# An attention and feed-forward kernel: everything that trails the scores is put one tile later

## The reference

```python
q_bits = (einsum('bhsd,dk->bhsk', q, proj) > 0)      # proj: 64 x 6, the same for k
mask   = q_bucket[..., :, None] == k_bucket[..., None, :]
scores = where(mask, q @ k.T / 8, -1e9)
attn   = exp(scores - rowmax) / (rowsum + 1e-9)
x = (attn @ v)                                       # 2 x 8 heads, 768 tokens, 64 wide -> 1536 x 512
h = x @ w_in;  g = 0 if h <= -1, h if h >= 1, (h+1)^2/4 between;  x = g @ w_out
h = x @ w_in2; g = h - tanh(h);                                   out = g @ w_out2
```

## Time and profile before

| | |
|---|---|
| median of 3 runs | 763.33 us (761.89 to 765.22) |
| the profiled execution | 763.58 us |
| its span, first to last instruction | 761.8 us |
| granted TensorE clock | 1.000 of full speed |
| first scores (pair 0, tile 0) | 7.35 us |
| last scores (pair 7, tile 11) | 224.62 us |
| first product of the second matrix of layer 1 | 249.00 us |

### The profile page before, as it was taken

One profiled execution on the slowest core, in us unless ns is written; L12 is line 12 of the kernel. 1 busy time (PEld: TensorE's weight loads), 2 busy tenths in 40 slices (PEclk: granted clock), 3 DMA queues, 4 the chain that ended last, 5 costly groups with the idle time before them and its releaser, 6 DMA issues.

```text
span 761.8 us, 11646 instructions
## 1 busy us (share of the span) xinstructions
PE 751.5 (99%) x3712; PEld 636.7 (84%) x3712; DVE 426.3 (56%) x741; ACT 343.3 (45%) x679; POOL 290.3 (38%) x226
## 2 busy tenths in 40 slices
PE   6999999999999999999999999999999999999998
PEld 4889989989998888888888888878888888888886
DVE  5999999999994674343433677762221322232223
ACT  5789788888894323343333323242221322222222
POOL 7667977977989992000000465650000000000000
PEclk9999999999999999999999999999999999999999
DMA  6545445454324131000000123210000100010001
GB/s 207 173 129 146 122 133 143 131 127 138 109 77 149 60 134 56 1 0 1 1 0 1 55 84 111 83 56 1 1 0 1 55 0 0 0 55 1 1 0 56
DMA packets 21032, 49.48 MB, mean 65 GB/s; under 512 B 4782, under 2 KB 6958, under 8 KB 21002
## 3 DMA queue, kind: packets, MB, share of 16 engines
q1 hardware_dynamic: 20858, 48.68, 21.2%
q10 hardware_dynamic: 144, 0.39, 0.1%
HBM read 41.26 MB, written 3.19 MB: 58 GB/s over the span
## 4 chain that ended last, share of the span: by engine, by line
PE 87%; DVE 8%; ACT 3%; issue 2%; DMA 0%; DVEq 0%; ACTq 0%
PE ps L677 29%; PE ps L598 29%; PE ps L589 9%; PE ps L575 9%; DVE g_raw L913 5%; PE ps L555 4%; PE ps L562 4%; PE ps L512 2%; DVE g_mid L910 1%; ACT g_mid L781 1%; ACT g_hi L787 1%; DMA qk_raw<-qk 0%; PE ps L519 0%; DVE clamped L836 0%; DVE g_lo L921 0%
## 5 line engine op out<-in xcount | busy, mean ns | idle before, releaser
L598 PE MATMUL ps<-x_hi,w 128*128 128x512 f32 (+1 forms) x768 | 251.8, 389 | 0.0
L921 DVE TENSOR_TENSOR g_lo<-g_raw,g_hi 128x512 fp32r<-128x512 f32 x96 | 71.1, 741 | 243.5 <-ACT g_hi L787 243.5
L787 ACT ACTIVATE g_hi<-g_raw 128x512 fp32r<-128x512 f32 x96 | 60.7, 632 | 289.0 <-PE ps L677 224.1
L598 PEld LDWEIGHTS ps<-x_hi,w 128*128 128x128 f32 x768 | 144.1, 188 | 29.7
L598 PE MATMUL ps<-x_lo,w 128*128 128x512 f32 (+1 forms) x384 | 149.4, 389 | 0.0
L677 PE MATMUL ps<-g_hi,w 128*128 128x512 f32 x384 | 125.8, 389 | 0.3 <-DVE g_lo L921 0.3
L677 PE MATMUL ps<-w,g_hi 128*128 128x512 f32 x384 | 118.2, 389 | 0.0
L853 DVE TENSOR_TENSOR p_lo<-ps,p_hi 128x384 fp32r<-128x384 f32 x192 | 97.9, 551 | 11.8 <-ACT p_hi L733 11.5
L373 POOL TENSOR_SCALAR w<-stage 128x1024 fp32r<-128x1024 f32 x32 | 37.8, 1180 | 163.8 <-PE ps L677 162.8
L733 ACT ACTIVATE p_hi<-ps 128x384 fp32r<-128x384 f32 x192 | 84.3, 488 | 30.6 <-PE ps L575 29.3
L723 ACT ACTIVATE probs<-clamped,row_stats 128x768 f32<-128x768 f32 x96 | 89.6, 933 | 6.9 <-DVE clamped L836 6.7
(11 more groups left out here) (62 smaller groups left out, 858.7 us busy)
## 6 DMA issues: line engine op xcount, KB each, us to landing
stage<-weights SPq DMA_DIRECT2D x32, 512.0 KB, 3.3
qk_raw<-qk SPq DMA_DIRECT2D x15, 384.0 KB, 4.2
q_raw<-qq SPq DMA_DIRECT2D x15, 384.0 KB, 4.2
k_raw<-kk SPq DMA_DIRECT2D x15, 384.0 KB, 5.1
v_raw<-v SPq DMA_DIRECT2D x16, 192.0 KB, 3.9
inv_wide<-factors SPq DMA_DIRECT2D x16, 192.0 KB, 4.2
out<-stage SPq DMA_DIRECT2D x12, 256.0 KB, 2.1
q_a<-q_b SPq DMA_DIRECT2D x14, 192.0 KB
```

What stands on the lines that cost most here:

```text
L598: last = nc.tensor.matmul(ps[:, f % H_BANKS, :], w[:, f, wp, k * P:(k + 1) * P], xs[:, k, bass.ds(t * TOK, TOK)], start=(k == 0 and wp == ...
L787: nc.scalar.activation(g_hi[:, slot, :], g_raw[:, slot, :], ACT.Copy).then_inc(g_hi_ready, 1)
L921: nc.vector.tensor_tensor(g_lo[:, slot, :], g_raw[:, slot, :], g_hi[:, slot, :].bitcast(F32), ALU.subtract).then_inc(g_split, 1)
```

## The change

Five constants grow by one tile, the two turns in which POOL scales become 9 and 11, and the two bit products move from the ends of turns 5 and 7 to the ends of turns 6 and 8, on PE and DVE alike. No instruction is added or removed.

```diff
-TRANSPOSE_LAG = 4
-PV_LAG = 8
-FOLD_LAG = 10
-FACTOR_LAG = 8
-SCALE_TURNS = [8, 10]
+TRANSPOSE_LAG = 5
+PV_LAG = 9
+FOLD_LAG = 11
+FACTOR_LAG = 9
+SCALE_TURNS = [9, 11]

-TURNS = [0, 1, 2, 3, 4, 5, "bits0", 6, 7, "bits1", 8, 9, 10, 11]
+TURNS = [0, 1, 2, 3, 4, 5, 6, "bits0", 7, 8, "bits1", 9, 10, 11]
 BITS_TURN = [TURNS.index("bits0"), TURNS.index("bits1")]
-BITS_AFTER = [5, 7]
+BITS_AFTER = [6, 8]
```

## The result

The changed kernel takes 769.23 us (median of 6 runs, 767.33 to 771.01), against 762.61 us for the kernel before (6 runs): 1.0084, with a 95% interval of 1.0067 to 1.0101. It is slower by 0.8%, 6.6 us in the medians. The profiled execution took 768.11 us, its span is 766.3 us, 4.5 us more than before.

A forecast was written before the change was run, and what follows sets the result against it. PE, busy 99%, was taken to bound the kernel, its stalls passed on in full. Losses of 1.2 + 1.3 + 3.4 = 5.9 us on 763.58 gave 769.5, or 769.2 against the median; stated 769.3, range 764.8 to 772.0.

The forecast's parts named there:

- pair 0 and its boundary, with the turn owed to the drain: Pair 0 with the deferred trailing turn in the drain loses 1.2 us; the boundary to pair 1 stalls 1.3 us.
- boundaries of pairs 1 to 6: Tile 0's scores wait for the copies at five boundaries, none at the last: 3.4 us in sum.
- The lags I cost at 0: Steady state of the attention: all trailing steps move together, so the longer lags cost 0.
- What doesn't move along: Tile 0's scores stay in turn 12 while bits1 ends a turn later, so PE waits for copies: 3.4 us.
- The bound from the store: Pair boundaries: the store behind the copies releases the spread, so copies land at most 7.65 us behind bits1; 4.4 us in sum.
- the cover: Time from the end of bits1 to tile 0's scores: 8.70 us before, 6.64 us after the change.
- The lower bound: Pair boundaries: DMA engines at 0.10 busy put the landing at least 6.5 us behind bits1; 0.2 us in sum.
- The rival of early copies: Copies land near the lower bound, leaving only the pinned tile and first boundary: 2 us, 765.4; chance 0.14.
- Pair 0: Bits0 falls behind tile 6, which waits for unmoved copies; tile 9 stays near 26.90, the drain adds 1.28: loss 1.2 us.
- tile 6 tied to 20.3: Pair 0: tile 6's scores wait for head 1's bits, which the change doesn't move, so they begin again at 20.3.
- The boundary to pair 1: End of pair 0: the chain takes 7.65 to 8.8 us, stalling tile 0 by 1.0 to 2.2 us, taken as 1.3.
- The rival "worse": Stalls delay the next threshold and loads, filling the queue: up to 0.7 us more per boundary, 10.8 us, 774.1; chance 0.05.

The follow-up runs named there:

- second profile: Profiled execution of the unmodified changed kernel run once more: 770.65 us, span 768.8 us; that run's median 770.85 us, ratio 1.0088 against the kernel before.
- before_filler: Kernel before plus 6 extra products of 384 columns, result unused, in pair 0's turn 5 between scores and transposes: 763.42 us, ratio 1.0001.
- Copies first: Changed kernel with SP's two 384 KB loads for the pair after next issued behind the three head 0 copies: 766.63 us, ratio 1.0060.
- bits alone: Kernel before with only the bit products and thresholds moved to the ends of turns 6 and 8, lags kept (also bits_only): 769.03 us, ratio 1.0086.
- both mends: Changed kernel with copies ahead of the loads and 11 extra products in pair 0 (also both_mended): 766.03 us, ratio 1.0026.
- Filler: Changed kernel with 11 extra products of 384 columns, result unused, on PE at the end of pair 0's turn 5: 767.48 us, ratio 1.0063.
- all_copies_first: Changed kernel with SP's copies ahead of the two loads everywhere, in pair 0 too, no product added: 767.41 us, ratio 1.0056.
- after_again: The changed kernel measured once more, unmodified, against the kernel before: 770.85 us (768.12 to 772.76), ratio 1.0088.

## Why the prediction was right

**The sum.** 769.3 was forecast and 769.23 measured, but so close a hit is luck. In us over the kernel before, the columns of the first and second profile against its own profile with the slower start, the last column against that of before_filler with the quicker one:

| | forecast | first profile | second profile | first, same start |
|---|---|---|---|---|
| pair 0 and its boundary, with the turn owed to the drain | 1.2 + 1.3 | 2.0 | 5.4 | 3.9 |
| boundaries of pairs 1 to 6 | 3.4 | 2.4 | 1.6 | 2.4 |
| pair 7, feed-forward | 0 | 0.1 | 0.1 | 0.1 |
| sum | 5.9 | 4.5 | 7.1 | 6.4 |

The second profile has the slower start too, so like is compared with like in the last two columns. There the later boundaries cost 1 to 2 us less than forecast and pair 0 1.4 to 2.9 more. The sum was near since the two errors offset.

**"The lags I cost at 0": half right.** In the changed kernel the steady turns are the 2.06, 2.20 and 2.30 us of before. But the reason given, that all steps move together, is what carries it: with the thresholds left behind the same lags cost 0.6 us a pair. And 0.15 us of each pair's loss is no copy's: it stays with the copies in time.

**"What doesn't move along": right in mechanism, too large in size.** The place, the waiting instruction and the cause were as forecast: tile 0's scores, waiting for the copies behind the moved threshold, at the ends of pairs 1, 4 and 5 and not of pair 6. Copies first takes the wait away, bits alone brings it about. Of 2.4 us in these pairs 1.7 is wait beyond 2.47 us a turn, where 3.4 was forecast; at two of the five boundaries (three in the second profile) there was no wait at all. The bound from the store was close in itself: where tile 0 waited, it came 0.04 to 0.09 us ahead of the spread. But from the end of bits1 to the spread it was 7.50, 6.57, 6.64, 7.04 and 7.75 us in this execution and 7.95, 7.60, 7.65, 7.21 and 7.22 in that of before, at equal distances of the issues. The landing differs from execution to execution, and the forecast took one execution's for fixed; the cover was 6.80 us and not 6.64, too. The lower bound was none: an engine share of 0.10 says that the data is through by then, not that it was on its way until then, and in pair 4 of bits_only the spread is issued 6.23 us behind bits1. The rival of early copies, which land 2.1 us behind the last issue, did not happen at the ends of pairs 1, 4 and 5: there PE waited until 3.1 to 3.8 us behind it.

**"Pair 0": the step that was incomplete.** "Bits0 stands behind tile 6 and only older transposes are left to fill" the wait is what happened. The turn owed to the drain also shows: with both mends pair 0 costs 0.2 us and the drain 1.4, where 1.2 was forecast for the two. What the forecast lacked is that the pause brings half clock behind it. That costs 1.6 us in the short case. In the long case PE's rows from tile 6 to tile 8 take 4.68 + 2.33 us where the filler's run has 2.43 + 1.58: 3.0 us. Filler and both_mended show that it is the clock; what makes a stretch short or long is open. It is not the length of the pause alone, since all_copies_first has the long stretch behind a pause of 2.04 us. Nor was tile 6 tied to 20.3; in the first profile it came at 18.40. That tile 9 came at 27.00, where about 26.90 was forecast, is a coincidence: the quicker start took 1.2 us off and the half clock put 1.6 on; in the second profile tile 9 came at 30.64. The boundary to pair 1 was taken as 1.3 us of wait. The last turn of pair 0 is 2.74 and 2.44 us in the two profiles and 2.06 with the copies first, so it was 0.7 and 0.4: the chain of 8.8 us in the trace of before came out as 7.1 and 6.8. The rival "worse", a queue that fills up from pair to pair, did not happen.

**The start.** Tile 6 comes at 18.4 to 18.5 us in the profiles of the changed kernel's versions with the quicker start, and at 20.3 and 20.7 in those of before and after_again with the slower one. Its copies wait for a threshold behind tile 2, so they move with the start: in the changed kernel the last of them is issued at 15.59 us in the first profile and at 17.26 in the second. Why an execution starts the one way or the other was not settled.

## What to carry to other kernels

When a step is moved in a written-out order, look for what it feeds that is not moved with it, and count the distance to that from its real chain: threshold, everything in the queue ahead, copy, landing. A DMA that somebody waits for should not be issued right behind large ones that nobody needs yet, even if its own issue comes no earlier for it; this order was harmless for as long as a turn of cover was left. A pause of PE can cost more than its length: time the work behind it at both clocks before calling the pause hidden. And before two executions are compared piece by piece, see whether they start alike.

## What the runs showed of the hardware

- A pause of PE of 2.0 us (0.37 us of work in 2 us) went with half clock, 1.2 GHz, from about 18.6 us to 22 us; another of 2.0 us (all_copies_first) with a stretch from 17.8 to 24.5; one of 2.6 us with one from about 20 to 26.5 us. The pause of 1.15 us in the kernel before left the clock at 1.00. All 12 runs of the changed kernel have a mean clock under 0.999; all 6 runs with the pause filled have 0.999 or 1.000, and so have all 12 with both mends. By the Trainium skill, "TensorE: Matmul & The Clock Gate", section "Part 1: The HAM clock gate", the gate follows PE's recent activity and has only these two levels. The rows agree: 0.50 or 1.00 in steps of half a microsecond, with something between only where the level changes.
- In some executions two products of 384 columns take 0.64 us at the start of the kernel and 0.35 us later, in others 0.35 from tile 1 on; the clock column reads 1.00 in either (before and after, 9 to 10.5 us).
- The same copies of 18 rows, issued at the same distances, let PE wait for 0 to 0.99 us from one pair to the next in one execution; with the two loads of 384 KB issued behind them and not ahead, for 0 in all, though the copies were issued no earlier.
